# Attention scores in quarters of the TensorE array, and a value product split by key halves

## The chip, the cores and the metric

One core of a Trainium2 chip. The metric is the device time of one execution in microseconds, the median of several runs.

## The reference, cut to what matters

Three stages follow one another. The first is gated linear attention for 4 sequences of 768 positions, 8 heads of 48 numbers; the second a top-2 mixture of 8 experts on the 3072 rows it gives; the third a gated two-layer block on all rows. Only the first is touched:

```
f = sigmoid(f_logit)
for t in range(768):
    state = f[t][:, None] * state + outer(k[t], v[t])   # per head, 48 x 48
    y[t] = q[t] @ state
```

## The kernel before

**Tiles.** The 3072 positions are 24 tiles of 128, worked on in 12 pairs, tiles a and b of a pair k. The tiles 0 to 5 are the first sequence, 6 to 11 the second, and so on. Within a tile the recurrence is turned into a causal product: y = (masked scores) times v, plus what the state brought from the tile before gives. The state is carried from tile to tile in a sequence; after the last tile of a sequence (the b of the pairs 2, 5, 8 and 11) there is none.

**Scores by levels.** Decay between a key and a query is worked in by six levels. Level 0 takes blocks of 4 positions, the levels 1 to 5 blocks of 8, 16, 32, 64 and 128, of which only the part with keys in the left half of a block and queries in its right half is new. `scores(t, n)` (L1827) computes level n of tile t on TensorE into the bank pair pA[t % 2]: for each of the 4 pairs of heads c, two matmuls, one for each head s, with the head's 64 rows as contraction, the tile's keys (128, later 112, 96, 64) as stationary columns and all 128 queries as moving columns. What isn't new is computed and thrown away. Then VectorE multiplies the scaled keys and queries W by products of decays in `double_blocks(t, n)` (L1315), which the next level's scores need. The new scores are taken to SBUF, into aT: levels 0 to 2 by VectorE, `take_masked` (L1338, a copy under a mask, over 1024 and then 512 elements a partition); levels 3 to 5 by ScalarE, `take_rect` (L985, rectangular blocks).

**Value product.** `attend(t, cs)` gives y of a tile: when a state is inherited, four matmuls of 128 by 128 (L1881) with it, then eight matmuls aT times v with all 128 keys (L1886). `turn_keys` (L1864) transposes the keys for the state, `key_values` (L1901) multiplies them with v, `turn_x` (L1911) transposes y, `logit_parts` (L1924), `logits` (L1934) and `ranks` (L1946) begin the routing of the second stage.

**Queues.** Every engine executes a queue written by hand, a `body(k)` for each pair. In body k TensorE computes the scores of pair k and the value products of pair k - 1 (tiles a - 2 and b - 2); other engines work on pair k + 1 too. The parts of the queues that matter here, in order:

- TensorE: the body that the diff shows.
- ScalarE: take_rect(b - 2, 5), take_logit_parts, take_keys(a - 2), take_keys(b - 2) unless b - 2 ends a sequence (L994, reads what turn_keys left), inner_decays(k + 1) (L963, L965), soft_noise (L1030 to L1038), take_y(a - 2) (L1000), decay_factors(k + 1) (L973, L974), spread_state(a - 2) (L1007), take_x(a - 2), take_rect(a, 3), take_rect(b, 3), take_y(b - 2), take_rect for level 4 and (a, 5), spread_state(b - 2), take_x(b - 2).
- GpSimd: decay_state(a - 2), add_noise (L767), clamp(k + 2) (L709), merge_inner(k + 1) (L719), turn_first for both tiles of pair k + 1 (L727, L728), products(k + 1) (L739, L744), decay_state(b - 2) (L752), four scatters (L776).
- VectorE: double_blocks(b - 2, 5), to_block_ends(b) (L1293), take_masked(a, 0), take_masked(b, 0), double_blocks(a, 1), take_masked(a, 1), take_ranks (L1433, waits for ranks and logits) and take_rows, double_blocks(b, 1), take_masked(b, 1), double_blocks(a, 2), take_masked(a, 2), new_state(a - 2) (L1347 or L1350), double_blocks(b, 2), take_masked(b, 2), top2 (L1385), double_blocks(a, 3), turn_others(a + 2) (L1283), double_blocks(b, 3), turn_others(b + 2), double_blocks(a, 4), two small steps, new_state(b - 2) (needs decay_state(b - 2)), double_blocks(b, 4), to_block_ends(a + 2), a small step, double_blocks(a, 5).

After the pairs, TensorE goes on to the experts (L2041, L2073) and the last stage (L2152). The first expert's weights are loaded by the sync queue once the last pair but one has its key_values(b - 2) (through load_v and its waits), and cast by ScalarE (L1055) in the middle of body 11.

## Time and profile before

| | |
|---|---|
| median of 3 runs | 1233.04 us (1231.67 to 1234.83) |
| span of the profiled execution | 1221.6 us |
| TensorE busy (matmul) | 1185.8 us, 97% of the span |
| VectorE, ScalarE, GpSimd busy | 687.1, 481.6, 479.4 us |
| attention pairs | from 0 to about 284 us |

The span is counted from the first to the last instruction; the profile gives no time of its own for what lies around it in that execution, and the median of the runs is 11.4 us above its span. The busy time of matmuls is modelled, so 97% doesn't say that TensorE is at its peak. A matmul on 32-bit data shows as two records.

### The profile page before, as it was taken

To read this page: it belongs to the slowest core of one execution; us is meant where nothing else is said; L and a number is where in the kernel's file an instruction comes from. 1 tells how busy PE (TensorE), PEld (TensorE's weight loads), DVE (VectorE), ACT (ScalarE), POOL (GpSimd) and SP (SyncE) were. 2 spreads that over 40 slices of the span, in tenths; PEclk is the share of its full clock that TensorE was granted. 3 is DMA by queue.
4 is the path that set the end of the run, shared out by engine and by line. 5 is a ranking of instruction groups with operands and counts; after the bars stand their busy time and mean duration, and the time that the engine had idled before them with its cause. 6 is when DMAs were issued, how large, how long until landed. Compare 5 with 4: busy or idle time off the path is not lost.

```text
span 1221.6 us, 25186 instructions
## 1 busy us (share of the span) xinstructions
PE 1185.8 (97%) x8085; PEld 1037.9 (85%) x8086; DVE 687.1 (56%) x1215; ACT 481.6 (39%) x968; POOL 479.4 (39%) x463
## 2 busy tenths in 40 slices
PE   4999999999999999999999999999999999999998
PEld 4777787788888999999999998888888888888887
DVE  7888988887534454544444554445445454454433
ACT  4666665556333343433333443332322323223212
POOL 8458777754573617163357552220020200100000
PEclk9999999999999999999999999999999999999999
DMA  6233343343577868687788864130030301201000
GB/s 229 72 112 122 123 140 101 109 167 124 188 234 236 250 199 260 202 255 224 237 248 267 248 221 145 52 104 27 28 77 26 104 27 45 60 26 52 27 1 26
DMA packets 109523, 164.78 MB, mean 135 GB/s; under 512 B 48384, under 2 KB 85504, under 8 KB 108928
## 3 DMA queue, kind: packets, MB, share of 16 engines
q1 hardware_dynamic: 97584, 115.48, 30.5%
q0 software_dynamic: 11712, 47.98, 12.6%
q8 instruction: 53, 0.87, 0.3%
q14 instruction: 30, 0.25, 0.1%
q10 hardware_dynamic: 144, 0.20, 0.0%
HBM read 107.45 MB, written 56.16 MB: 134 GB/s over the span
## 4 chain that ended last, share of the span: by engine, by line
PE 82%; POOL 6%; DVE 4%; issue 3%; ACT 2%; DMA 2%; SPq 0%; DVEq 0%; POOLq 0%; ACTq 0%
PE pD L2041 17%; PE pD L2152 12%; PE pA L2152 12%; PE pA L2073 9%; PE pS L2073 9%; PE pA L2180 6%; PE pA L1850 5%; PE pX L2180 3%; PE pS L2180 3%; DVE W L1315 1%; POOL qk L728 1%; POOL fT L709 1%; POOL prods L744 1%; DMA stage<-w 1%; POOL qk L727 1%
## 5 line engine op out<-in xcount | busy, mean ns | idle before, releaser
L2041 PE MATMUL pD<-we,xsH 128*128 x612 | 189.6, 391 | 0.1
L1850 PE MATMUL pA<-W 64*128 64x128 f32 (+3 forms) x1920 | 136.8, 283 | 15.7 <-DVE W L1315 12.2
L1763 DVE TENSOR_TENSOR gs<-pD,sig 128x512 f32<-128x512 f32 x71 | 49.1, 692 | 169.3 <-ACT sig L1229 169.3
L1850 PEld LDWEIGHTS pA<-W 64*128 64x128 f32 (+3 forms) x1920 | 112.7, 170 | 34.8 <-DVE W L1315 18.7
L948 POOL DMA_INDIRECT pair<-y_sorted,y_row x40 | 38.8, 970 | 248.9 <-DMA z_rows<-pair 229.5
L2041 PEld LDWEIGHTS pD<-we,xsH 128*128 128x128 f32 x612 | 114.1, 188 | 22.2 <-issue 0.5
L2041 PE MATMUL pD<-we,xsL 128*128 x306 | 120.1, 392 | 0.0
L1229 ACT ACTIVATE sig<-pD 128x512 f32<-128x512 f32 x71 | 42.6, 600 | 192.4 <-PE pA L2152 192.4
L1315 DVE TENSOR_TENSOR W<-W,prods 128x512 f32<-128x512 f32 (+1 forms) x120 | 101.9, 856 | 22.9 <-PE pA L1850 20.8
L2073 PE MATMUL pA<-we,hidH 128*128 (+1 forms) x448 | 114.5, 336 | 0.0
L1495 DVE STREAM_TRANSPOSE pA<-hidP 128x512 f32<-128x512 f32 x98 | 64.6, 705 | 81.5 <-DMA hidP<-hid_rows 81.3
L2073 PE MATMUL pS<-we,hidH 128*128 x416 | 106.1, 336 | 0.4 <-ACT yo L1136 0.4
L1128 ACT ACTIVATE hidH<-pA 128x512 fp32r<-128x512 f32 x110 | 65.1, 599 | 95.0 <-DVE pA L1495 91.4
L837 POOL TENSOR_TENSOR we<-stage,we 128x1536 fp32r<-128x1536 f32 x28 | 98.6, 3521 | 0.6
L1487 DVE STREAM_TRANSPOSE pX<-xs 128x384 f32<-128x384 f32 x50 | 35.6, 712 | 104.4 <-DMA xs<-x_sorted 104.2
L1122 ACT ACTIVATE hid<-pD 128x512 f32<-128x512 f32 x100 | 59.9, 600 | 82.9 <-PE pD L2041 74.3
L2152 PE MATMUL pA<-zH,valL 128*128 128x512 f32 x216 | 85.9, 399 | 0.0
L2152 PE MATMUL pD<-zH,gateL 128*128 128x512 f32 x216 | 85.9, 399 | 0.0
L2152 PE MATMUL pD<-zH,gateH 128*128 128x512 f32 x216 | 85.6, 398 | 0.0
L1235 ACT CAST uH<-u 128x512 fp32r<-128x512 f32 x71 | 44.1, 620 | 105.3 <-DVE u L1766 103.8
L2152 PE MATMUL pA<-zH,valH 128*128 128x512 f32 x216 | 84.8, 394 | 0.0
L2152 PE MATMUL pA<-zL,valH 128*128 128x512 f32 x216 | 84.4, 392 | 0.0
(315 smaller groups left out, 2660.9 us busy)
## 6 DMA issues: line engine op xcount, KB each, us to landing
hid_rows<-hid SPq DMA_DIRECT2D x49, 512.0 KB, 3.4
hidP<-hid_rows SPq DMA_DIRECT2D x196, 128.0 KB, 2.9
stage<-w POOLq DMA_DIRECT2D x48, 384.0 KB, 4.7
qk<-qk_t SPq DMA_DIRECT2D x24, 512.0 KB, 3.7
y_sorted<-yo SPq DMA_DIRECT2D x53, 192.0 KB
xs<-x_sorted SPq DMA_DIRECT2D x200, 48.0 KB, 2.1
fT<-f_t SPq DMA_DIRECT2D x12, 512.0 KB, 4.2
vN<-v_n SPq DMA_DIRECT2D x24, 256.0 KB, 2.7
```

The source lines that it names most:

```text
L837: return pool.tensor_tensor(low, src, high.bitcast(F32), ALU.subtract)
L1122: act.activation(to, fr, ACT.Relu).then_inc(s_relu, 1)
L1128: act.activation(hidH[t.par][:, h * HF:(h + 1) * HF], pA[0][:, h], ACT.Relu).then_inc(s_hh, 1)
L1235: act.copy(uH[f % 2][:], u[f % 2][:]).then_inc(s_uh, 1)
L1315: dve.tensor_tensor(half[:, used], half[:, used], other[:, used], ALU.mult).then_inc(s_upd[t % 2], 1)
L1495: dve.transpose(pA[0][:, h].rearrange("p (k j t) -> p k j t", k=k, j=Q), hidP.rearrange("p (j k f) -> p k j f", j=Q, k=FC)[:, h * k:(h + 1 ...
L1763: dve.tensor_tensor(gs[:], pD[:, f % 2 * 512:f % 2 * 512 + TT], sig[f % 2][:], ALU.mult).then_inc(s_u, 1)
L1850: ins = pe.matmul(pA[par][keys, s, c * P:(c + 1) * P], both[r, 1, c, keys], both[r, 0, c], start=True, stop=True)
L2041: ins = pe.matmul(hidden_bank(t, h), (xsL if a else xsH)[t.par][:, k * P:(k + 1) * P], we[:, bass.ds(at + (b * WE + k * F + h * HF), HF)], ...
L2073: ins = pe.matmul(y_bank(t), (hidL if a else hidH)[t.par][:, k * P:(k + 1) * P], we[:, bass.ds(at + ((2 + b) * WE + k * DM), DM)], start=k ...
L2152: ins = pe.matmul(bank, (low if b else high)[:, c:c + P], (zL if a else zH)[t.par][:, k * TT:(k + 1) * TT], start=n == 0, stop=n == len(or ...
L2180: ins = pe.matmul(out_bank(j), (uL if a else uH)[f % 2][:, j * P:(j + 1) * P], outL[:, f * DM:(f + 1) * DM] if b else high[:, at * DM:(at ...
```

## The change

The scores of a level are no longer computed with 128 queries for all keys. For levels 0 to 4 each head gets two matmuls, left keys by left queries and right keys by right queries, 64 by 64 each, so four quarters of the array (two heads by two key halves) are addressed with 64 moving columns. Level 5 has left keys by right queries alone. A head's scores now take 64 columns in PSUM, and take_masked reads half as many elements. The two tiles' scores of a level stand next to each other in TensorE's queue. The value product is cut in three: `inherit` (the state's part, now eight matmuls of 64 output rows), `attend_late` (late keys, by late queries only; it needs level 4 at most) and `attend` (the first 64 keys, all queries). turn_keys(b - 2), ranks and logits come after attend(a - 2). The masks get three more copies at the start on GpSimd. The queues of the other engines keep their order.

```diff
...
 
 def block_masks(pool, mask, done):
 
+    lower = slice(HS, P)
     for l, h in enumerate(SMALL):
         v = mask[:, l * HP * HS:(l + 1) * HP * HS].rearrange("p (c b u) -> p c b u", c=HP, u=h)
         nb = P // (2 * h)
         pool.affine_select(out=v, in_=v, pattern=[[0, HP], [-2 * h, nb], [0, h]], compare_op=ALU.is_ge,
                            fill=0.0, base=0, channel_multiplier=1).then_inc(done, 1)
-        pool.wait_ge(done, 2 * l + 1)
+        pool.wait_ge(done, 3 * l + 1)
         pool.affine_select(out=v, in_=v, pattern=[[0, HP], [2 * h, nb], [0, h]], compare_op=ALU.is_ge,
                            fill=0.0, base=h - 1, channel_multiplier=-1).then_inc(done, 1)
-        pool.wait_ge(done, 2 * l + 2)
+        pool.wait_ge(done, 3 * l + 2)
+        pool.tensor_copy(v[lower, :, 0:nb // 2], v[lower, :, nb // 2:]).then_inc(done, 1)
+        pool.wait_ge(done, 3 * l + 3)
     n = len(SMALL)
     v = mask[:, n * HP * HS:].rearrange("p (b u) -> p b u", u=BASE)
 
     pool.affine_select(out=v, in_=v, pattern=[[-BASE, P // BASE], [0, BASE]], compare_op=ALU.is_ge,
                        fill=0.0, base=0, channel_multiplier=1).then_inc(done, 1)
-    pool.wait_ge(done, 2 * n + 1)
+    pool.wait_ge(done, 3 * n + 1)
     pool.affine_select(out=v, in_=v, pattern=[[BASE, P // BASE], [1, BASE]], compare_op=ALU.is_ge,
                        fill=0.0, base=0, channel_multiplier=-1).then_inc(done, 1)
+    pool.wait_ge(done, 3 * n + 2)
+    pool.tensor_copy(mask[lower, n * HP * HS:n * HP * HS + HS],
+                     mask[lower, n * HP * HS + HS:n * HP * HS + P]).then_inc(done, 1)
+    pool.wait_ge(done, 3 * n + 3)
 
 
 def halves_of(pair, h):
...
                 h = LEVELS[n - 1]
                 for b in range(P // (2 * h)):
                     left = slice(2 * h * b, 2 * h * b + h)
-                    right = slice(2 * h * b + h, 2 * h * (b + 1))
-                    ins = act.copy(aT[t % 4][left, :, :, right],
-                                   pA[t % 2][left].rearrange("p s (c n) -> p s c n", c=HP)[:, :, :, right])
+                    at = 2 * h * b % HS + h
+                    fr = pA[t % 2][left, :, 0:HP * HS].rearrange("p s (c n) -> p s c n", c=HP)
+                    if n < NL:
+                        fr = fr[:, :, :, at:at + h]
+                    ins = act.copy(aT[t % 4][left, :, :, at:at + h], fr)
                 ins.then_inc(s_rect[t % 2], 1)
 
             def take_keys(t):
...
                 i = t // 2
                 dve.wait_ge(s_a[t % 2], FILLS * i + n + 1)
                 if n == 0:
-                    dve.wait_ge(s_cs, 2 * MASKED)
+                    dve.wait_ge(s_cs, 3 * MASKED)
                     if t >= 4:
                         dve.wait_ge(s_y, t - 3)
                 else:
                     dve.wait_ge(s_lev[t % 2], MASKED * i + n)
+                to = aT[t % 4][:, :, :, 0:HS].rearrange("p a c b -> p (a c) b")
+                fr = pA[t % 2][:, :, 0:HP * HS].rearrange("p a (c b) -> p a c b", b=HS)
                 if n:
                     h = LEVELS[n - 1]
-                    to = aT[t % 4].rearrange("p a c (b s u) -> p a (c b) s u", s=2, u=h)[:, :, :, 1]
-                    fr = pA[t % 2].rearrange("p a (b s u) -> p a b s u", s=2, u=h)[:, :, :, 1]
+                    to = to.rearrange("p m (b s u) -> p m b s u", s=2, u=h)[:, :, :, 1]
+                    fr = fr.rearrange("p a c (b s u) -> p a c b s u", s=2, u=h)[:, :, :, :, 1]
                     at = (n - 1) * HP * HS
-                    mk = mask[:, at:at + HP * HS].rearrange("p (b u) -> p b u", u=h)
-                    mk = mk.unsqueeze(1).to_broadcast([P, 2, HP * HS // h, h])
+                    mk = mask[:, at:at + HP * HS].rearrange("p (c b u) -> p c b u", c=HP, u=h)[:, 0, 0:HS // (2 * h)]
+                    mk = mk.unsqueeze(1).to_broadcast([P, H, HS // (2 * h), h])
                 else:
-                    to = aT[t % 4].rearrange("p a c b -> p (a c) b")
-                    mk = mask[:, len(SMALL) * HP * HS:].unsqueeze(1).to_broadcast([P, H, P])
-                    fr = pA[t % 2].rearrange("p a (c b) -> p (a c) b", b=P)
+                    at = len(SMALL) * HP * HS
+                    mk = mask[:, at:at + HS].unsqueeze(1).to_broadcast([P, H, HS])
                 dve.copy_predicated(to, mk.bitcast(I32), fr).then_inc(s_lev[t % 2], 1)
 
             def new_state(t):
...
                     else:
                         pe.wait_ge(s_rect[par], RECTS * i + n - MASKED)
                 both = W[t % 6] if n else qk[t % 4]
+                left, right = slice(0, HS), slice(HS, P)
+                blocks = ((left, right),) if n == NL else ((left, left), (right, right))
                 for c in range(HP):
-                    for s in range(2):
-                        r = slice(HS * s, HS * (s + 1))
-                        keys = slice(0, P - LEVELS[n - 1] if n >= MASKED else P)
-                        ins = pe.matmul(pA[par][keys, s, c * P:(c + 1) * P], both[r, 1, c, keys], both[r, 0, c],
-                                        start=True, stop=True)
+                    for keys, asks in blocks:
+                        for s in range(2):
+                            r = slice(HS * s, HS * (s + 1))
+                            ins = pe.matmul(pA[par][keys, s, c * HS:(c + 1) * HS], both[r, 1, c, keys],
+                                            both[r, 0, c, asks], start=True, stop=True)
                 ins.then_inc(s_a[par], 1)
 
             def turn_keys(t):
...
                     ins = pe.transpose(pX[:, c * P:(c + 1) * P], W[t % 6][:, 1, c], ident[:])
                 ins.then_inc(s_kt, 1)
 
-            def attend(t, cs):
+            def inherit(t):
 
                 pe.wait_ge(s_upd[t % 2], NL * (t // 2 + 1))
-                pe.wait_ge(s_rect[t % 2], RECTS * (t // 2 + 1))
+                pe.wait_ge(s_yt, t)
+                pe.wait_ge(s_spread, states_up_to(t - 1))
+                for c in range(HP):
+                    for s in range(2):
+                        pe.matmul(pD[HS * s:HS * (s + 1), c * P:(c + 1) * P], stateB[1 - t % 2][:, c, s],
+                                  W[t % 6][:, 0, c], start=c == 0, stop=False, skip_group_check=True)
+
+            def attend_late(t):
+
+                pe.wait_ge(s_rect[t % 2], RECTS * (t // 2) + RECTS - 1)
                 pe.wait_ge(s_v[t % 4], 16 * (t // 4 + 1))
                 if t == 0:
                     pe.wait_ge(s_clear, 1)
                 else:
                     pe.wait_ge(s_yt, t)
-                inherits = not first_of_sequence(t)
-                if inherits:
-                    pe.wait_ge(s_spread, states_up_to(t - 1))
-                if inherits and cs[0] == 0:
-                    for c in range(HP):
-                        pe.matmul(pD[:, c * P:(c + 1) * P], stateB[1 - t % 2][:, c].rearrange("p s d -> p (s d)"),
-                                  W[t % 6][:, 0, c], start=c == 0, stop=False, skip_group_check=True)
-                for c in cs:
-                    y = pD[:, c * P:(c + 1) * P]
+                late = slice(HS, P)
+                for c in range(HP):
                     for s in range(2):
-                        ins = pe.matmul(y[HS * s:HS * (s + 1)], vN[t % 4][:, 2 * c + s], aT[t % 4][:, s, c],
-                                        start=not inherits, stop=True, skip_group_check=True)
-                if cs[-1] == HP - 1:
-                    ins.then_inc(s_y, 1)
+                        ins = pe.matmul(pD[HS * s:HS * (s + 1), c * P + HS:(c + 1) * P], vN[t % 4][late, 2 * c + s],
+                                        aT[t % 4][late, s, c, 0:HS], start=first_of_sequence(t) and c == 0,
+                                        stop=False, skip_group_check=True)
+                ins.then_inc(s_late, 1)
+
+            def attend(t):
+
+                pe.wait_ge(s_rect[t % 2], RECTS * (t // 2 + 1))
+                pe.wait_ge(s_late, t + 1)
+                soon = slice(0, HS)
+                for c in range(HP):
+                    for s in range(2):
+                        ins = pe.matmul(pD[HS * s:HS * (s + 1), c * P:(c + 1) * P], vN[t % 4][soon, 2 * c + s],
+                                        aT[t % 4][soon, s, c], start=False, stop=True, skip_group_check=True)
+                ins.then_inc(s_y, 1)
 
             def key_values(t):
 
...
                 now, old = is_pair(k), is_pair(p)
                 if now:
                     scores(a, 0)
+                    scores(b, 0)
                 if old:
                     turn_keys(a - 2)
+                    if not first_of_sequence(a - 2):
+                        inherit(a - 2)
                 if now:
-                    scores(b, 0)
+                    scores(a, 1)
+                if old:
+                    attend_late(a - 2)
+                if now:
+                    scores(b, 1)
+                if old:
+                    attend(a - 2)
                 if old and not last_of_sequence(b - 2):
                     turn_keys(b - 2)
-                if now:
-                    scores(a, 1)
                 if is_pair(k - 3):
                     ranks(k - 3)
                 if is_pair(k - 2):
                     logits(k - 2)
                 if old:
-                    attend(a - 2, (0,))
-                if now:
-                    scores(b, 1)
-                if old:
-                    attend(a - 2, (1, 2, 3))
+                    key_values(a - 2)
                 if now:
                     scores(a, 2)
-                if old:
-                    key_values(a - 2)
-                if now:
                     scores(b, 2)
                 if old:
                     turn_x(a - 2)
+                    inherit(b - 2)
                 if now:
                     scores(a, 3)
                 if old:
-                    attend(b - 2, (0,))
+                    attend_late(b - 2)
                 if now:
                     scores(b, 3)
                 if old:
-                    attend(b - 2, (1, 2, 3))
-                if now:
-                    scores(a, 4)
+                    attend(b - 2)
                 if old and not last_of_sequence(b - 2):
                     key_values(b - 2)
                 if now:
+                    scores(a, 4)
                     scores(b, 4)
-                if now:
-                    scores(a, 5)
                 if old:
                     turn_x(b - 2)
                 if now:
+                    scores(a, 5)
                     scores(b, 5)
                 if old:
                     logit_parts(p)
...
             turn_keys(a)
             ranks(NP - 3)
             logits(NP - 2)
-            attend(a, (0,))
+            inherit(a)
+            attend_late(a)
             turn_rows(Tile(0))
-            attend(a, (1, 2, 3))
+            attend(a)
             key_values(a)
             hidden(Tile(0))
             pe.wait_ge(s_xl, 1)
             turn_x(a)
-            attend(b, (0, 1, 2, 3))
+            inherit(b)
+            attend_late(b)
+            attend(b)
             turn_hidden(Tile(0))
             logit_parts(NP - 1)
             turn_x(b)
```

## Rows read from the trace of the kernel before

**Rows 1.** The page: busy time of TensorE, and the chain by engine.

```profile
PE 1185.8 (97%) x8085; PEld 1037.9 (85%) x8086; DVE 687.1 (56%) x1215; ACT 481.6 (39%) x968; POOL 479.4 (39%) x463
...
PE 82%; POOL 6%; DVE 4%; issue 3%; ACT 2%; DMA 2%; SPq 0%; DVEq 0%; POOLq 0%; ACTq 0%
```

**Rows 2.** Busy time by stretch of 30 us (from:to, length, engines).

```profile
150.00:180.00 30.00, 28.89 (x394) 24.13 (x392) 26.14 (x54) 18.55 (x44) 21.51 (x27) 1.00 0.46 143
...
330.00:360.00 30.00, 30.00 (x154) 26.95 (x153) 9.43 (x15) 9.58 (x19) 26.12 (x18) 1.00 0.70 200
```

**Rows 3.** Groups of instructions by line, 60 to 330 us.

```profile
L1850 PE MATMUL pA<-W 64*128 64x128 f32 (+3 forms) x1584 | 112.0, 281 | 10.8 <-DVE W L1315 9.6 <-DVE aT L1338 1.1
...
L1338 DVE COPY_PREDICATED aT<-mask,pA 128x512 f32<-128x512 int32 (+1 forms) x58 | 51.5, 895 | 0.9 <-PE pA L1850 0.9
```

**Rows 4.** Timeline of TensorE (start, length, what): logit_parts, right behind scores(b, 5).

```profile
54.63 0.64 PE L1924 MATMUL pD<-yT,wr 128*32 128x256 f32 x8
...
77.79 0.64 PE L1924 MATMUL pD<-yT,wr 128*32 128x256 f32 x8
...
100.78 0.64 PE L1924 MATMUL pD<-yT,wr 128*32 128x256 f32 x8
...
123.81 0.64 PE L1924 MATMUL pD<-yT,wr 128*32 128x256 f32 x8
...
147.31 0.64 PE L1924 MATMUL pD<-yT,wr 128*32 128x256 f32 x8
...
169.79 0.64 PE L1924 MATMUL pD<-yT,wr 128*32 128x256 f32 x8
```

**Rows 5.** The chain, 99.8 to 122.8 us (start, length, what).

```profile
99.83 1.02 PE pA L1850 x16
...
104.19 0.60 PE pX L1864 x4
...
104.81 0.59 ACT kEnd L994
...
108.18 0.23 POOL rsp L767
...
121.18 0.47 POOL stateD L752
...
122.05 0.69 DVE W L1315
```

**Rows 6.** The chain in pair 10, where TensorE alone carries it.

```profile
245.14 0.37 PE pD L1886 x4
245.51 1.09 PE pA L1850 x16
246.60 0.81 PE pD L1886 x12
...
248.50 0.60 PE pS L1901 x16
```

**Rows 7.** Timeline of VectorE, 122 to 169 us.

```profile
126.22 2.48 DVE L1338 COPY_PREDICATED aT<-mask,pA 128x1024 f32<-128x1024 int32 x2
...
162.30 1.16 DVE L1315 TENSOR_TENSOR W<-W,prods 128x512 f32<-128x512 f32 x1
...
167.38 0.71 DVE L1315 TENSOR_TENSOR W<-W,prods 128x512 f32<-128x512 f32 x1
```

**Rows 8.** Timeline of the start: TensorE and GpSimd.

```profile
12.90 2.08 PE L1850 MATMUL pA<-qk 64*128 64x128 f32 x16 [12.90 <-POOL qk L728]
...
9.51 1.04 POOL L719 TENSOR_TENSOR FG<-FG 128x512 f32<-128x512 f32 x1 [1.64 <-ACT FG L974]
```

**Rows 9.** The chain at the end of the pairs.

```profile
258.72 12.03 DMA stage<-w
```

**Rows 10.** Between the stages: timeline of TensorE, then its busy time and granted clock.

```profile
762.35 1.09 PE L2192 MATMUL pX<-ident,z_first 128*128 128x128 f32 x4 [2.14 <-DVE z_first L1784]
...
763.00:764.00 1.00, 1.00 (x6) 0.50 0.00 0
```

More of the change, by code:

```diff
@@ L365, in program @@
         s_y = sem("s_y")
+        s_late = sem("s_late")
         s_yt = sem("s_yt")
```

## The prediction

> **What bounds the kernel now.** I read the page first: TensorE is busy 97% and holds 82% of the chain [rows 1]. That is an average over stages, so I cut the span by time. In the expert stages TensorE is busy 30.00 us of 30; in the attention pairs it is 28.89 and VectorE 26.14, so neither is simply the bound [rows 2]. The change touches only the pairs, up to some 284 us. There the scores cost 112.0 us of TensorE and the masked copies 51.5 us of VectorE [rows 3]: both get cheaper, and that is the tempting sum. So I looked at what closes the loop from pair to pair. The end of a pair is its logit_parts: the pairs 2 to 6 take 23.16, 22.99, 23.03, 23.50 and 22.48 us [rows 4]. The chain of pair 4 [rows 5] is to be read as a ring: scores(b, 5) at 99.83, then TensorE up to the end of turn_keys(b - 2) at 104.79, ScalarE (take_keys, inner_decays, soft_noise) to 108.18, GpSimd from add_noise through clamp, merge, turn_first and products to decay_state, ending at 121.65, VectorE (new_state, double_blocks(b, 4)) to 122.74, and TensorE's next scores(b, 5). 4.96 + 3.4 + 13.5 + 1.1 = 23.0 us. Where tile b - 2 has a state to pass on (pairs 1, 2, 4, 5, 7, 8) this ring sets the period; where it has none (pairs 3, 6, 9) TensorE and VectorE do, hand in hand.
>
> **What a matmul costs.** In [rows 6] twelve records take 0.81 us and four take 0.37: the eight more are four slots of two heads, 0.11 us a slot, and 0.15 us is left, which I read as the change from one shape of the array to another. With 64 stationary and 48 moving columns sixteen records take 0.60: less 0.15, 0.056 a slot. Quarters of 64 by 64 with 64 moving columns never ran. If all four of a group share a slot, scores take 8 x 0.058 = 0.46 us, 0.61 with a change of shape, against 1.09. If only two quarters run at a time it is 16 x 0.058 + 0.15 = 1.08. I take the first: two row halves share a slot in the scores of before, two column halves in attend. No row shows both at once; the bounds are 0.46 and 1.08.
>
> The Trainium skill (TensorE: Matmul & The Clock Gate, on the back-to-back issue gap) has matmuls start no closer than some 25 ns. By that the 32 records of a quartered score would take 0.8 us in place of 0.46. No row here shows small quarters; the sum does without it.
>
> **The change part by part.**
>
> *TensorE.* inherit: eight matmuls of two records, 8 x 0.11 + 0.15 = 1.03, as before. attend_late: new, 8 x 0.058 = 0.46 between scores of the same shape. attend: 0.88 + 0.15 with its change, less 0.15 where scores of the same shape precede: 0.88. Two tiles' scores together: 0.92 + 0.15 = 1.07. A pair's work on TensorE falls by some 12 x 0.5 - 0.9 = 5 us.
>
> *VectorE.* The level 0 copy goes from 1024 to 512 elements, 1.24 [rows 7] to about 0.7 (the mixed mean of both sizes is 0.895 [rows 3]), the others from 0.7 to 0.4: 2 x 0.6 + 4 x 0.3 = 2.4 us a pair.
>
> *Where turn_keys(b - 2) goes.* It now stands behind scores(a, 1), attend_late, scores(b, 1) and attend of a - 2. Behind it in ScalarE's queue stand take_keys(b - 2), inner_decays, soft_noise, take_y and decay_factors, and GpSimd's whole part of the ring waits for them. From scores(b, 5): 0.46, logit_parts 0.6, both level 0 scores 1.07, turn_keys(a - 2) 0.6, inherit 1.03, together 3.8 us. scores(a, 1) needs take_masked(a, 0): VectorE reaches it 3.5 us after double_blocks(b, 4) (126.22 [rows 7] less 122.74 [rows 5]) and needs 0.7, so it starts at 4.3. Then 0.46, 0.46, 0.46, 0.88 and turn_keys 0.6: 7.2 us against 4.96, 2.3 later. The GpSimd part shrinks from 13.5 to some 12.7, since decay_factors is then ready in time and VectorE's operations overlap it less (bounds 12.0 and 13.5). Ring: 7.25 + 3.4 + 12.7 + 1.1 = 24.45 us. Against before: pairs 4 and 7 +1.4 each, 2, 5 and 8 +1.1 each, together +6.1. Pair 1 has no soft_noise to wait for; its decay_factors was behind attend alone and is now behind turn_keys and inner_decays: +2.0.
>
> *Pairs 3, 6, 9.* No turn_keys(b - 2). attend ends at 6.6, ranks and logits at 7.6; take_ranks and take_rows now hold VectorE until 8.4, double_blocks and the copy of (b, 1) end at 9.5, (a, 2) and new_state at 11.3, spread_state at 12.0, inherit(b - 2) at 13.1, scores(a, 3) at 13.7. From there the old stretch of double_blocks and turn_others, 162.30 to 168.0 [rows 7], 5.7 us: 19.4 in place of 22.7. 3 x 3.3 = -9.9 us.
>
> *Filling, pair 0.* TensorE and VectorE alternate. The halved copies give 2.4 us, and some four waited-for scores 0.5 each, more while the first still take 2.08 [rows 8] (twice the 1.09 of later): -4.3. The mask copies: three short ones, nothing longer than GpSimd's affine steps of the same size, in the 1.64 us that GpSimd waits for ScalarE [rows 8]; hidden, and if the cover is gone they cost at most what exceeds it.
>
> *Pairs 10 and 11, and the end.* The load of the first expert starts behind key_values(b - 2) of pair 10 and takes 12.03 us [rows 9]; ScalarE waits for it in body 11. key_values comes 0.4 us sooner, and half of pair 11 behind that wait is shorter by 0.8: -1.2. Behind the pairs two attend_late (0.9) and VectorE's work, which no longer hides behind TensorE (0.8): +1.7.
>
> Without the clock: -4.3 + 6.1 + 2.0 - 9.9 - 1.2 + 1.7 = -5.6 us.
>
> *The clock.* TensorE has 5 us less to do in a ring that is 1 us longer. In the ring pairs its idle time gathers in two places: before inherit(b - 2), which waits for spread_state behind decay_factors (some 2.5 us), and before scores(b, 5) (some 3.5 us). The longest such gap in the pairs now is 1.4. What a longer one does, the trace shows once: TensorE sat idle for 2.14 us, and behind it the granted clock was 0.50, that is 1.2 GHz, until 766 us [rows 10], some 3.4 us. The gap before scores(b, 5) lies just ahead of the 7.2 us of the ring that are TensorE's. If the clock falls there, 2.6 us of path at full clock cost 1.3 more. Eight pairs (1, 2, 4, 5, 7, 8, 10, 11): +10.4. I take it, because both gaps are longer than the one that did it. Bounds: 0 and, if the whole 7.2 us ran slow, of which half is waiting for VectorE, 8 x 3 = 24.
>
> The Trainium skill (the same page, its table on why this matters) asks for no long idle gaps between bursts of matmuls, else the clock halves. By that the sum is 10.4 us above the one without gaps, as I took it from the rows; the trace agrees with its one fall.
>
> Sum: -5.6 + 10.4 = +4.8. The sum is made against the span of 1221.6, which becomes 1226.4; with the 11.4 us between span and median, 1238.
>
> **The rivals.**
>
> A. *The clock holds.* For it: a single fall in the trace, at a place where the matmuls before were of another kind; the gaps of 1.4 us did nothing. Then 1233.0 - 5.6 = 1227.4 us, faster. It decides if gaps of 2.5 and 3.5 us leave the clock at 2.4 GHz.
>
> B. *Quarters run two at a time.* Then scores cost as before: seven of a ring pair's stand on the path or in inherit's, and TensorE is the bound: +0.5 us for four scores in the ring (2.0 a pair, 8 pairs) and 2.5 in the others, some +24, while the busy TensorE keeps its clock (-10): 1252 us.
>
> C. *The ring isn't rigid.* GpSimd could make up the delay, if its part shrinks towards what its operations take alone and new_state isn't last. Then all pairs gain like 3, 6 and 9: 11 x 3.3 + 4.3 = 40 us less, 1193. Against it: at 121.65 VectorE starts new_state in the same tenth of a microsecond as decay_state ends [rows 5].
>
> **How the numbers follow.** Less than 0.3% (3.7 us) can't be told from no change here. Forecast (ring longer, clock falls) 45%, its own range 1230 to 1248; A 30%, 1220 to 1233; B 17%, 1243 to 1264; C 8%. From the forecast 0.30 lies above 1236.7, 0.15 within; A gives 0.08 within and 0.22 below; B is all slower, C all faster. Together slower 0.47, same 0.23, faster 0.30. From 1222 to 1256, C, the low end of A and the high end of B are left out, two in ten.
>
> **What would show it.** Ring: logit_parts to logit_parts 24 to 26 us in the pairs 1, 2, 4, 5, 7, 8, under 21 in 3, 6, 9. Scores: sixteen matmuls, 32 records, in about 0.5 to 0.6 us. take_keys(b - 2) ends 7 to 9 us behind scores(b, 5) instead of 5.6. Clock: below 1.00 in windows of the pairs. VectorE: copies at some 0.7 and 0.4 us. I'd be wrong if GpSimd's idle time before add_noise grew without the pair's period growing, or if scores stayed near 1.09.

## The result and the profile after

The changed kernel takes 1271.1 us (median; 1262.5 to 1273.9), the kernel before 1232.4 beside it: ratio 1.030, interval 1.028 to 1.033. The forecast was 1238, 1222 to 1256: the direction was right, the time lay outside the range. The profiled execution has a span of 1267.5 us, 46.0 more than before, and a mean granted clock of 0.957.

The page after: TensorE's busy time, its granted clock in the 40 slices, the instruction queue, the chain by engine.

```profile
PE 1174.8 (93%) x10549; PEld 1030.1 (81%) x10550; DVE 656.0 (52%) x1215; ACT 478.3 (38%) x968; POOL 483.7 (38%) x466
...
PEclk9886796888999999999999999999999999999999
...
q8 instruction: 72, 1.18, 0.4%
...
PE 75%; POOL 7%; issue 5%; DMA 5%; DVE 3%; ACT 3%; SPq 1%; DVEq 0%; POOLq 0%; ACTq 0%
```

TensorE is busy 11 us less than in [rows 1], though part of its work ran at half clock, and it waits more; every digit of the clock below 9 lies in slices 2 to 10, among the attention pairs. Windows of TensorE (columns as in [rows 2]):

```profile
150.00:180.00 30.00, 22.71 (x620) 19.61 (x622) 20.85 (x48) 17.52 (x47) 24.22 (x27) 0.89 0.27 99
...
101.00:108.00 7.00, 6.29 (x112) 4.72 (x116) 6.58 (x11) 1.95 (x5) 6.12 (x8) 0.51 0.03 11
108.00:111.40 3.40, 2.18 (x63) 1.64 (x64) 0.15 (x1) 0.54 (x1) 2.58 (x3) 1.00 0.42 164
111.40:125.00 13.60, 12.50 (x190) 11.04 (x187) 6.19 (x25) 6.68 (x15) 6.08 (x8) 0.50 0.36 114
```

The last row shows a whole pair's middle at 1.2 GHz: 13.6 us at 0.50. In all, 109 us of the first 345 are at half clock; in the kernel before none. The costliest group of the pairs, against [rows 3]:

```profile
L1863 PE MATMUL pA<-W 64*64 64x64 f32 x2880 | 88.0, 247 | 38.7 <-DVE W L1325 24.9 <-DVE aT L1349 7.6 <-issue 6.1
```

The scores of levels 1 to 5 take 88.0 us, part of them at half clock, where they took 112.0, and the idle time ahead of them has grown from 10.8 to 38.7 us. The logit_parts on the timeline, as in [rows 4]:

```profile
56.52 0.64 PE L1950 MATMUL pD<-yT,wr 128*32 128x256 f32 x8
...
81.75 1.08 PE L1950 MATMUL pD<-yT,wr 128*32 128x256 f32 x8
...
103.88 1.08 PE L1950 MATMUL pD<-yT,wr 128*32 128x256 f32 x8
...
133.81 1.08 PE L1950 MATMUL pD<-yT,wr 128*32 128x256 f32 x8
...
163.53 1.08 PE L1950 MATMUL pD<-yT,wr 128*32 128x256 f32 x8
...
185.43 0.64 PE L1950 MATMUL pD<-yT,wr 128*32 128x256 f32 x8
```

The same eight matmuls take 0.64 or 1.08 us: the second is the half clock at the end of pairs 2 to 5. The differences of such starts are the periods of the pairs, here for this and for later kernels (us; last column: us at half clock in the first 345):

| pair | 2 | 3 | 4 | 5 | 6 | 7 | 8 | 9 | 10 | 11 | half |
|---|---|---|---|---|---|---|---|---|---|---|---|
| before | 23.2 | 23.0 | 23.0 | 23.5 | 22.5 | 23.0 | 23.5 | 22.5 | 22.7 | 22.6 | 0 |
| after | 25.2 | 22.1 | 29.9 | 29.7 | 21.9 | 30.0 | 29.9 | 21.9 | 28.2 | 28.4 | 109 |
| fill | 24.4 | 21.3 | 29.8 | 26.7 | 22.0 | 29.1 | 27.1 | 22.1 | 28.5 | 30.4 | 61 |
| fill_more | 24.4 | 22.7 | 24.0 | 25.2 | 23.0 | 24.8 | 24.8 | 21.0 | 23.6 | 26.4 | 20 |
| keys_ranks_fill | 21.9 | 20.7 | 21.4 | 22.4 | 20.2 | 21.4 | 22.4 | 23.8 | 21.3 | 31.3 | 20 |
| quarters_old_order | 23.8 | 19.9 | 24.6 | 24.3 | 21.5 | 24.3 | 27.4 | 21.0 | 25.8 | 23.2 | 58 |
| quarters_old_order_fill | 22.0 | 21.0 | 23.3 | 21.6 | 21.3 | 21.6 | 22.0 | 20.7 | 20.6 | 22.6 | 3 |
| before_fill | 25.0 | 24.1 | 24.4 | 25.4 | 24.1 | 24.4 | 25.4 | 24.1 | 24.7 | 25.4 | 0 |
| before_wait | 24.1 | 23.3 | 22.8 | 26.1 | 23.5 | 22.8 | 24.5 | 26.0 | 25.4 | 24.3 | 14 |

The chain after, in pair 4, to be laid beside [rows 5]:

```profile
102.83 1.12 PE pA L1863 x16
103.95 1.01 PE pD L1950 x8
104.96 1.92 PE pA L1863 x64
106.88 1.04 PE pX L1877 x4
107.92 0.67 PE pA L1863 x32
...
112.71 1.69 PE pD L1913 x16
114.40 1.06 PE pX L1877 x4
115.48 0.59 ACT kEnd L1004
...
118.76 0.23 POOL rsp L775
...
131.16 0.47 POOL stateD L760
...
132.03 0.69 DVE W L1325
132.72 0.04 issue
132.77 1.12 PE pA L1863 x16
```

It is the forecast ring: scores(b, 5), TensorE to the end of turn_keys(b - 2), ScalarE, GpSimd, VectorE, scores(b, 5). But TensorE's part takes 115.46 - 102.83 = 12.6 us, where 7.2 were forecast. The rest is 3.3 + 12.9 + 1.1, as forecast.

### The profile page after: what moved, and what is told of

It reads as the page before. It is cut to its first block, busy times and chain, and to the rows that moved or that the text cites. A ratio compares the mean times of both kernels' runs of the same rounds, so it can differ in the third digit from the quotient of the medians.

```text
span 1267.5 us, 30091 instructions
## 1 busy us (share of the span) xinstructions
PE 1174.8 (93%) x10549; PEld 1030.1 (81%) x10550; DVE 656.0 (52%) x1215; ACT 478.3 (38%) x968; POOL 483.7 (38%) x466
## 3 DMA queue, kind: packets, MB, share of 16 engines
q0 software_dynamic: 11712, 47.98, 11.9%
## 4 chain that ended last, share of the span: by engine, by line
PE 75%; POOL 7%; issue 5%; DMA 5%; DVE 3%; ACT 3%; SPq 1%; DVEq 0%; POOLq 0%; ACTq 0%
PE pD L2066 14%; PE pA L2180 12%; PE pD L2180 12%; PE pA L2098 8%; PE pS L2098 7%; PE pA L2208 6%; PE pA L1863 4%; PE pX L2208 3%; PE pS L2208 3%; DMA hidP<-hid_rows 2%; DMA hid_rows<-hid 2%; DVE W L1325 1%; PE pD L1913 1%; POOL qk L736 1%; POOL prods L752 1%
## 5 line engine op out<-in xcount | busy, mean ns | idle before, releaser
L1863 PE MATMUL pA<-W 64*64 64x64 f32 x3456 | 107.1, 254 | 45.3 <-DVE W L1325 26.6
L1863 PEld LDWEIGHTS pA<-W 64*64 64x64 f32 x3456 | 88.8, 161 | 61.0 <-DVE W L1325 38.9
L2066 PEld LDWEIGHTS pD<-we,xsH 128*128 128x128 f32 x612 | 114.1, 188 | 23.2 <-issue 1.3
L1325 DVE TENSOR_TENSOR W<-W,prods 128x512 f32<-128x512 f32 (+1 forms) x120 | 92.5, 779 | 58.0 <-PE pA L1863 43.9
L2180 PE MATMUL pD<-zL,gateH 128*128 128x512 f32 x216 | 84.4, 392 | 0.0
```

The source lines that it names most:

```text
L1325: dve.tensor_tensor(half[:, used], half[:, used], other[:, used], ALU.mult).then_inc(s_upd[t % 2], 1)
L1863: ins = pe.matmul(pA[par][keys, s, c * HS:(c + 1) * HS], both[r, 1, c, keys], both[r, 0, c, asks], start=True, stop=True)
L2066: ins = pe.matmul(hidden_bank(t, h), (xsL if a else xsH)[t.par][:, k * P:(k + 1) * P], we[:, bass.ds(at + (b * WE + k * F + h * HF), HF)], ...
L2180: ins = pe.matmul(bank, (low if b else high)[:, c:c + P], (zL if a else zH)[t.par][:, k * TT:(k + 1) * TT], start=n == 0, stop=n == len(or ...
```

## The experiments

Theory 1: the order makes the ring longer, as forecast, and the clock takes the rest. Rivals: stalls in TensorE's supply of instructions (theory 2); the order costs all of it (theory 3).

**fill.** Dummy matmuls in two places of the ring pairs; they wait as scores(t, n) does until its PSUM is free.

```diff
+                    if now and not last_of_sequence(b - 2):
+                        fill(a, 3, 5)
                     inherit(b - 2)
...
+                    if old and not last_of_sequence(b - 2):
+                        fill(b, 5, 10)
                     scores(b, 5)
+            def fill(t, n, times):
...
+                for _ in range(times):
+                    pe.matmul(pA[par][:, 0, 0:P], ident[:], ident[:], start=True, stop=True)
```

> The changed kernel with matmuls added that do no useful work: five of 128 by 128 before inherit(b - 2) and ten before scores(b, 5), in the pairs whose tile b - 2 has a state to pass on, where TensorE waits anyway. Theory (ring and clock): the ring stays as it is, but TensorE stays at 2.4 GHz; ring pairs take about 24.6 us instead of 29.8, the mean granted clock is 0.99 or more, and the time is about 1233 us (1227 to 1240). Rival 1 (the new order of the queue alone makes the pair long and the clock costs little): 1265 us or more. Rival 2 (the small matmuls themselves, or fetching so many instructions, cost the time): 1270 us or more, since there are more instructions still.

Measured: 1264.1 us, ratio 1.027; a miss by 31 us. The half clock fell to 61 us and pairs 5 and 8 lost 3 us, pairs 4 and 7 little, since their clock still fell. Too few dummies to decide.

**full_new_order.** The new order with the scores, masks and copies of the kernel before.

> The new order of TensorE's queue and the value product by key halves, but with the scores of before: all 128 queries, masks and copies of before. Theory: TensorE is busy, so the clock holds (0.99 or more), but turn_keys(b - 2) ends 9.9 us behind scores(b, 5), so a ring pair takes about 27.5 us and the time is about 1262 us (1250 to 1275). Rival 1: the same. Rival 2 (small matmuls are the cost): near 1235 us.

Measured: 1266.6, ratio 1.030. The pairs 4, 5, 7 and 8 take 27.2, 26.9, 27.1 and 26.9 us with no half clock in them. The order and the value product in three parts cost some 4 us a ring pair when the scores are at full price.

**quarters_old_order.** All new matmuls, masks and copies, with the queue order of before (attend(a - 2, ...) replaced by inherit, attend_late and attend at its two places).

> All new matmuls, masks and copies, but TensorE's queue in the order of before (inherit and attend_late where attend of the first head pair stood). Theory: turn_keys(b - 2) ends 3.5 us behind scores(b, 5); the ring falls to about 21 us and TensorE is busy enough to keep its clock for the most part (0.98 or more): about 1207 us (1200 to 1222). Rival 1: faster too. Rival 2 (small matmuls are the cost): 1245 us or more.

Measured: 1239.7, ratio 1.007; a miss by 33 us. Without any new order the clock falls too, 58 us in all, and the cheaper matmuls give nothing.

**keys_ranks_early.** The changed kernel with both turn_keys side by side, and ranks and logits behind scores(a, 1).

```diff
                     turn_keys(a - 2)
+                    if not last_of_sequence(b - 2):
+                        turn_keys(b - 2)
                     if not first_of_sequence(a - 2):
                         inherit(a - 2)
```

> The changed kernel with three steps moved back: turn_keys(b - 2) right behind turn_keys(a - 2), ranks and logits right behind scores(a, 1). The adjacent scores stay. Theory: turn_keys(b - 2) ends 3.8 us behind scores(b, 5), the ring is about 21 us, and the gaps that slow the clock go: about 1208 us (1200 to 1225). Rival 1 (adjacent scores are what costs): 1250 us or more. Rival 2 (small matmuls are the cost): 1250 us or more.

Measured: 1246.5, ratio 1.013; a miss again, by 38 us, with 68 us at half clock. These two kernels lay 33 and 38 us above their expectations, with 58 and 68 us at half clock: the clock had to be tested by itself.

**fill_more.** As fill, with more dummies and in every pair.

```diff
-                    if now and not last_of_sequence(b - 2):
-                        fill(a, 3, 5)
+                    if now:
+                        fill(a, 3, 9 if not last_of_sequence(b - 2) else 4)
...
+                        fill(b, 4, 3 if not last_of_sequence(b - 2) else 5)
...
+                        fill(a, 5, 3 if not last_of_sequence(b - 2) else 4)
...
+                        fill(b, 5, 9 if not last_of_sequence(b - 2) else 4)
```

> The changed kernel with more dummy matmuls (128 columns, identity by identity, into PSUM that the next scores overwrite; they compute nothing that is used): behind the copy of level 3 of tile a 9 in pairs that follow a pair of the same sequence on the state chain and 4 in the others, ahead of scores(b,4) 3 and 5, ahead of scores(a,5) 3 and 4, ahead of scores(b,5) 9 and 4. Theory 1 (the clock alone makes the difference between the forecast period and the measured one): half-speed time falls from 109 us of the changed kernel to under 15 us, pairs 4, 5, 7, 8 take 24.5 to 25.5 us instead of 30, pairs 10 and 11 25 instead of 28.3, the whole 1238 to 1245 us. Theory 2 (the stalls in which TensorE's records are 0.4 us apart have a cause of their own, the supply of its instructions): the clock still falls in several pairs, they stay at 27 or above, and the whole is 1255 or more. Theory 3 (order costs 4 us a pair by itself, as with full-width scores): the clock holds and the pairs still take 27: 1255.

Measured: 1237.2, ratio 1.008 (1.007 to 1.010). Work was added and 34 us came back; by the ratios it is 27, since the kernel before took 1226.1 beside this run and 1232.4 beside the changed kernel. That lies at the lower edge of theory 1's range, with 20 us at half clock where under 15 were expected. Its chain in pair 4:

```profile
103.25 0.64 PE pA L1863 x16
...
106.52 0.69 PE pA L1863 x32
...
108.95 0.60 PE pX L1877 x4
109.57 0.58 ACT kEnd L1004
...
112.86 0.23 POOL rsp L775
...
125.53 0.47 POOL stateD L760
```

TensorE's part is 6.3 us instead of 12.6. The pairs 2, 4, 5, 7 and 8 take 24.4, 24.0, 25.2, 24.8 and 24.8: on average 24.6, at full clock in all five, where the forecast ring without the clock was 24.45. At the end of pair 7 the chain runs through the dummies themselves (2.21 us from 198.01 on), so 24.6 is rather too long for the ring.

**quarters_old_order_fill** (fill(b, 4, 3 or 4), fill(a, 5, 3 or 4), fill(b, 5, 6 or 4) in quarters_old_order) and **keys_ranks_fill** (the same and fill(a, 3, 5 or 3) in keys_ranks_early).

> All matmuls, copies and masks of the changed kernel in the order of the kernel before, with dummy matmuls (128 columns, nothing of them is used) ahead of scores(b,4), scores(a,5) and scores(b,5): 3 or 4, 3 or 4, 6 or 4 of them. Without them this order had 58 us at half clock and took 1239.7. Theory 1 (clock alone): the half-speed time falls under 10 us; each us at half clock costs about half a us of the matmuls in it, so 20 to 28 us come back: 1212 to 1222, faster than before. Theory 2 (instruction supply): stalls and half clock stay in pairs 4, 7 and 9: 1232 to 1242.

> The changed kernel with turn_keys(b-2) right behind turn_keys(a-2) and ranks and logits right behind scores(a,1), and dummy matmuls (nothing of them is used) behind the copy of level 3 of tile a and ahead of scores(b,4), scores(a,5), scores(b,5). Without them it took 1246.5 with 68 us at half clock. Theory 1 (clock alone): clock above 0.99, ring pairs 22.5 to 23.5, the others 20.3 to 21: 1212 to 1222. Theory 2 (instruction supply): pair 5 stays near 30, whole 1238 to 1248.

Measured: 1211.1, ratio 0.987 (0.985 to 0.990), and 1217.1, ratio 0.992. The first lies just under theory 1's range, the second within it. The first is the fastest kernel of this study: the change's matmuls are worth 1.3% once TensorE is kept busy, and 3% against the kernel before with the same dummies (before_fill, below). In its chain a tile's scores take what was forecast:

```profile
117.03 0.61 PE pA L1863 x16
117.64 0.57 PE pD L1950 x8
118.21 0.62 PE pA L1863 x32
118.84 0.60 PE pX L1877 x4
```

keys_ranks_fill has one pair of 31.3 us; its timeline and its windows there:

```profile
247.46 1.08 PE L1863 MATMUL pA<-qk 64*64 64x64 f32 x57
250.59 0.39 PE L1863 MATMUL pA<-qk 64*64 64x64 f32 x7 [2.05 <-issue]
```

```profile
250.80:267.90 17.10, 16.33 (x229) 14.49 (x222) 6.50 (x25) 6.43 (x13) 3.08 (x6) 0.50 0.34 120
268.00:275.00 7.00, 7.00 (x207) 6.32 (x207) 4.91 (x8) 4.19 (x14) 3.42 (x4) 1.00 0.30 117
```

In the midst of one block of scores TensorE stands still for 2.05 us without waiting for an engine, and behind it the clock is 0.50 for 17.1 us, with 13 records a microsecond instead of 30. A pause as in theory 2 comes first and half clock as in theory 1 follows; that the one brings the other is not shown. The only fall in the pairs of quarters_old_order_fill, at 107.6 us, also stands right behind such a pause, of 1.79 us.

**split_moving.** The kernel before with each score matmul cut in two, but for the last level (so levels 0 to 4; the expectation misnames them), to add instructions alone.

```diff
-                        ins = pe.matmul(pA[par][keys, s, c * P:(c + 1) * P], both[r, 1, c, keys], both[r, 0, c],
-                                        start=True, stop=True)
+                        for q in range(1 if n == NL else 2):
+                            asks = slice(0, P) if n == NL else slice(HS * q, HS * (q + 1))
+                            at = c * P + asks.start
+                            ins = pe.matmul(pA[par][keys, s, at:at + asks.stop - asks.start], both[r, 1, c, keys],
+                                            both[r, 0, c, asks], start=True, stop=True)
```

> The kernel before with each score matmul of levels 0 to 7 cut into two of 64 moving columns: same order, same weights loaded twice, same values, and over 2000 more TensorE instructions, as the change adds. The scores of a tile are expected at 1.0 to 1.3 us. Theory 1 (clock alone): as before where they cost the same, 1228 to 1236, no half clock; if a score of a tile rises to 1.3 us it is up to 0.2 x 16 a pair dearer: 1240 to 1250, with each pair longer by the same amount. Theory 2 (instruction supply): idle pieces of 0.4 us between groups of 4 to 6 TensorE records and waits on remote semaphores of VectorE of 3 to 5 us appear that the kernel before doesn't have, and the clock falls in those pairs: 1240 or more, with some pairs longer by 2 to 7 us and others by nothing.

Measured: 1340.0, ratio 1.093. A tile's scores took 2.05 us, not 1.0 to 1.3, so TensorE became the bound and the comparison with theory 2 is weak: no remote wait and no idle piece, but no fast bursts either. What it says of columns stands at the end.

**before_fill.** The control: the kernel before with the dummies of quarters_old_order_fill.

> The kernel before with the dummy matmuls of the run quarters_old_order_fill (13 or 12 of 128 columns a pair, nothing of them is used), so a control: what the dummies cost or give where the clock was full anyway. They stand on TensorE's stretch, of which only the two ring parts set the period. The clock theory, in which they do nothing but hold the clock: 0 to +0.7 us a pair (13 x 0.056 where TensorE's work is the limit), 1226 to 1234, ratio 1.000 to 1.006. If dummies helped in some other way than by the clock (by spacing out the stalls), this kernel would get faster too, below 0.997.

Measured: 1246.8, ratio 1.018 (1.016 to 1.019), 13 us above what was expected at most. The dummies cost 1.8 us a pair where the clock was full anyway, so what they brought in fill_more is net of a price. But the kernel before has no stalls either (no idle piece that waits for nothing, 30 to 345 us). So this control doesn't tell whether the dummies help by holding the clock alone or by keeping the stalls away too, and no run separates the two.

**keys_early_fill.** keys_ranks_fill with ranks and logits left where the change has them.

> The changed kernel with turn_keys(b-2) alone moved, right behind turn_keys(a-2) (ranks and logits stay behind), and dummy matmuls (nothing of them is used) that hold the clock. It asks which step of the ring the order lengthened. If it is the place of turn_keys(b-2), as forecast (2.5 us more of the ring): ring pairs at full clock 22 to 22.8 us against 24.4 of fill_more and 21.4 to 22.4 of keys_ranks_fill, whole 1215 to 1225. If the place of ranks and logits counts as much (they feed pick and the noise on VectorE, which stand in the ring), ring pairs stay at 23.5 or more: 1228 to 1236.

Measured: 1227.6, ratio 1.002. Pairs 4, 5, 7 and 8 take 23.2, 24.1, 23.4 and 24.1, between the two cases: against fill_more (average 24.7) the keys give 1.0 and, against keys_ranks_fill (21.9), ranks and logits 1.8 more. Each of these pairs has 3.4 us at half clock, which may be most of the 1.8. Pair 2 is at full clock in all three kernels and takes 24.4, 23.4 and 21.9: 1.0 for the keys (with a few dummies less), 1.5 for the logits (there are no ranks yet in pair 2). Its chain in keys_early_fill passes from attend through the logits (L1960, 59.13) to ScalarE's soft_noise (59.72) and GpSimd's add_noise (60.48). Both steps of the order lengthen a pair, and I had counted only the first.

**old_order_keys_fill.** quarters_old_order_fill with turn_keys(b - 2) straight behind turn_keys(a - 2).

> The run quarters_old_order_fill (1211.1, ratio 0.9874) with turn_keys(b-2) straight behind turn_keys(a-2) instead of behind scores(b,0). If the ring (scores(b,5), turn_keys(b-2), ScalarE's copy, GpSimd, VectorE) still sets every ring pair, its TensorE part gets shorter by scores(b,0), 0.5 to 0.6 us, in seven ring pairs: 1206 to 1209. If VectorE's level chain of the two tiles sets the period there (its waits for TensorE's scores are 24 us over the stage), scores(b,0) comes later by 0.6 us and the same is lost: 1210 to 1215.

Measured: 1214.5, ratio 0.991: no gain. In that kernel the ring no longer sets the period alone.

**before_wait.** The kernel before with one more wait.

```diff
                 if old:
+                    if now:
+                        pe.wait_ge(s_lev[1], MASKED * (b // 2 + 1))
                     turn_x(a - 2)
```

> The kernel before, every instruction and its order kept, with one more wait on TensorE: ahead of turn_x(a-2) it waits until VectorE and ScalarE have copied level 2 of tile b. By the trace of before this makes TensorE idle from 135.93 to 137.98, 2.05 us, in every pair from 2 on, of which later idle pieces (0.39 and 0.59 us) and the slack of the stretch can take back about 1. If an idle piece of 2 us is by itself enough to lose the clock: half clock appears in most pairs, 3 to 14 us each, none in the unchanged kernel, and the time is 20 to 60 us longer: 1246 to 1286; if the 0.4 us pieces and the remote waits come with the half clock and not from the number of instructions, they appear here too, with the instructions of the kernel before. If the clock falls in the changed kernel for another reason (quarters, more instructions), it stays at full here and each pair takes 1 us more at most: 1226 to 1237.

Measured: 1241.1, ratio 1.015 (1.011 to 1.020), between the two cases. Two of its eleven waits on the timeline, and three windows behind them:

```profile
93.92 0.65 PE L1911 MATMUL pX<-ident,yT 128*128 128x128 f32 x4 [2.10 <-DVE aT L1338]
...
140.62 0.65 PE L1911 MATMUL pX<-ident,yT 128*128 128x128 f32 x2 [2.10 <-DVE aT L1338]
```

```profile
94.00:98.00 4.00, 4.00 (x48) 3.36 (x48) 3.20 (x8) 1.51 (x5) 3.92 (x6) 1.00 0.02 4
...
140.70:144.10 3.40, 3.40 (x22) 2.82 (x23) 1.42 (x7) 0.84 (x3) 3.25 (x6) 0.50 0.00 0
144.20:148.00 3.80, 3.80 (x53) 3.20 (x54) 2.37 (x4) 2.02 (x9) 3.41 (x6) 1.00 0.02 4
```

The same 2.10 us of idle time are followed by full clock once and by half clock the other time; of eight idle pieces of 2.1 us three were, in pairs 5, 9 and 10 (the other three were of 1.4 to 1.5 us, and none of them was). So the clock can fall at such an idle piece, with no quarter and no instruction added, but does not always, and it stays low for 3.4 to 6.8 us. Pairs 5 and 8, which took 23.5 both before, take 26.1 with 3.4 us at half clock and 24.5 without: 1.6 us for 3.4. There are no 0.4 us stalls and no remote waits here.

**old_order_fill_less.** quarters_old_order_fill with 7 dummies a pair.

> The run quarters_old_order_fill (1211.1, ratio 0.9874, 3.4 us at half clock) with 7 dummy matmuls a pair instead of 13 or 12: 2 ahead of scores(b,4), 2 ahead of scores(a,5), 3 ahead of scores(b,5). The dummies cost the kernel before 1.7 us a pair. If fewer still hold the clock, 0.3 to 0.8 us a pair come back: 1203 to 1208. If the clock falls in some pairs, each us at half clock costs about 0.5: 20 us of it give 1215 to 1222.

Measured: 1211.8, ratio 0.988. Half the dummies, four falls of 3.4 us instead of one, and the time is between the two cases: what one gives the other takes.

## Why the prediction was wrong

The span grew by 46.0 us and not by 4.8. (Between the medians it is 38.7 us: the profiled execution of the kernel before lay 11.4 us under its median, that of the changed kernel 3.6, so some 7 us of the 46.0 come from which executions were profiled.) Where the 41.2 lie, from the starts of logit_parts:

| part | forecast | measured | missed |
|---|---|---|---|
| filling and pair 1 (-4.3 + 2.0 + 1.3) | -1.0 | +1.9 | 2.9 |
| pairs 2, 4, 5, 7, 8 (+6.1 + 5 x 1.3) | +12.6 | +28.5 | 15.9 |
| pairs 3, 6, 9 | -9.9 | -2.1 | 7.8 |
| pairs 10, 11 (-1.2 + 2 x 1.3) | +1.4 | +11.4 | 10.0 |
| end | +1.7 | +2.9 | 1.2 |
| expert stages and last stage | 0 | +3.4 | 3.4 |

*Scores and copies: right.* 0.61 to 0.62 us in the chain against the forecast 0.61; rival B is out. The Trainium skill (TensorE: Matmul & The Clock Gate, the back-to-back issue gap) lets matmuls start no closer than some 25 ns, from which the estimate was 0.8 us: 0.62 for 32 records is 19 ns each, so the measurement decides against that estimate for quarters. VectorE's copies, by their line:

```profile
L1349 DVE COPY_PREDICATED aT<-mask,pA x60: 416/430/740, 59.6 to 309.6; 128x256 f32<-128x256 int32 x40, 128x512 f32<-128x512 int32 x20
```

0.43 and 0.74 us, forecast 0.4 and 0.7.

*The ring: right in size, in part by luck.* It carries the chain, it is rigid (rival C is out), and at full clock it takes 24.6 us in fill_more against 24.45. But the forecast put the whole lengthening down to turn_keys(b - 2), of which keys_early_fill shows some 1.0 us; the logits, which it had not counted in the ring, make 1.5. Pair 2 of the changed kernel, whose TensorE part ran at full clock, has 7.5 us from scores(b, 5) to the end of turn_keys(b - 2), forecast 7.2.

*The clock: the mis-sized term, and the step that failed.* "If the clock falls there, 2.6 us of path at full clock cost 1.3 more" took one fall of 3.4 us a ring pair, as the one of [rows 10]. (As it is worded the sum doesn't come out: 2.6 us of path at full clock would cost 2.6 more. 1.3 is the price of 2.6 us spent at half clock.) With it TensorE's part of the ring would have been 7.2 + 1.3 = 8.5 us. Measured are 12.6, 11.9, 12.2 and 12.1 us in the pairs 4, 5, 7 and 8, some 5 us above 7.2 in each. Two things make them.

The first is the half clock itself: falls of 3.4 to 13.7 us, two in each of the ring pairs 2, 4, 5, 7 and 8, 109 us in all. In pairs 5 and 8, 9.4 and 9.7 us of TensorE's part ran at 0.50. Even the bound of 24 us (3 us a pair) was too low. The idle pieces were there (1.96 us before scores(b, 5) at 132.77, 2.44 and 3.11 us before others), shorter than the forecast 3.5. The mistake was to carry over the length of the only low stretch, which lies in another stage. Why the clock stays low for longer in the pairs is not shown: idle time alone doesn't explain it, since in the 13.6 us shown above TensorE was busy 12.50 us.

The second is a term that the sum did not have: stalls, idle pieces of some 0.4 us in which TensorE waits for nothing that the profile shows, in the pairs 4, 7, 10 and 11. They are shown under "What stays open". From scores(a, 1) to the end of turn_keys(b - 2) pair 4 takes 7.5 us and pair 7 takes 8.0, against 3.0 in fill_more (from 106.52 to 109.55). Of these 4.5 and 5.0 us some 1.2 are half clock on attend and turn_keys; the other 3.3 and 3.8 are the stalls and the short pieces between them, at full clock for the most part. All idle pieces that wait for nothing add up to 11.0 us between 30 and 345 us in the changed kernel, to 2.9 in fill_more and to none in the kernel before.

Together: the four pairs 4, 5, 7 and 8 take 29.9 on average, with 15.1 us at half clock, and 24.7 in fill_more, 5.2 us a pair, 0.34 for each microsecond at half clock with the stalls counted in. Over 109 us that is an estimate of 37, against the 10.4 in the sum: some 27 of the 41 missed, for clock and stalls together and rough in size. The Trainium skill (TensorE: Matmul & The Clock Gate, on why this matters) asks for no long idle gaps between bursts; this case agrees in part: in before_wait it is a risk at each gap and not a rule, and split_moving lost the clock with no gap at all.

*Pairs 3, 6, 9: forecast too short by 1 us or more, clock or not.* Forecast 19.4. In the changed kernel pairs 6 and 9 take 21.9 with 2.5 and 2.7 us at half clock. Half clock can cost at most half of its own length, here 1.4 us, so 20.5 is left. The fill kernels of the new order agree, with 20.2 (keys_ranks_fill) and 21.0 (fill_more, pair 9) at the shortest. So less than two thirds of the expected 3.3 us was there, and the clock took part of that.

*The filling* had 10.2 us at half clock before 50 us, which the sum did not have at all, and its gain of 4.3 was eaten: the first logit_parts starts at 56.52, against 54.63 before. In keys_ranks_early, with full clock up to there, it starts at 52.05.

*What stays open.* 3.4 us in the stages behind the pairs. And stalls that appear after and not before: pieces in which TensorE runs five or six records and stops.

```profile
109.68 0.35 PE L1863 MATMUL pA<-W 64*64 64x64 f32 x4
110.43 0.35 PE L1863 MATMUL pA<-W 64*64 64x64 f32 x5 [0.40 <-issue]
111.18 0.36 PE L1863 MATMUL pA<-W 64*64 64x64 f32 x6 [0.41 <-issue]
111.95 0.76 PE L1863 MATMUL pA<-W 64*64 64x64 f32 x17 [0.41 <-issue]
```

They stand ahead of the 13.6 us at half clock, while the clock is still 1.00, and also at 190, 272 and 313 us: the first three times in the dense run of quarters behind turn_keys(a - 2), the last time behind inherit(b - 2). In the chain of pair 7 the stretch from scores(a, 1) to the end of turn_keys(b - 2), with the stalls of 190 us in it, goes from the first of these lines to the end of the second:

```profile
189.01 0.69 PE pA L1863 x32
...
195.99 1.06 PE pX L1877 x4
```

Waits of VectorE and ScalarE on no engine of the core appear as well:

```profile
DVE W L1325 <- remote: 14.2, 4, 5.2
...
ACT aT L996 <- remote: 5.2, 1, 5.2
```

Such waits occur in after, fill, full_new_order, quarters_old_order and keys_ranks_early, which have 17 to 109 us at half clock; all of these but full_new_order also have the stalls in series. Neither the waits nor the series occur in the kernels with more instructions still but enough dummies, nor in split_moving with 68 us at half clock. So neither the added instructions nor the half clock make them alone. Whether the stalls are late instructions that low clock and idle time bring about, or the other way round, no run settles.

## What to carry to other kernels

Making TensorE's work cheaper in a loop whose period another chain sets turns it into idle time, and this idle time can cost the clock: here matmuls worth 1.3% ended, by the new order, the clock and the stalls, as a loss of 3%. Read the granted clock in windows of one period, not on the page; and before moving or shaving anything test the kernel with dummy matmuls where the gaps would be, which separates the order from the rest if there are enough of them (those of fill were too few), and run the kernel before with them too, for their price. Where a step is moved behind others, count every consumer that it feeds: here the places of turn_keys and of ranks and logits each cost a ring pair one to two microseconds.

## What the hardware showed

- Halving the moving columns alone saves nothing. In split_moving:

```profile
116.82 2.05 PE L1853 MATMUL pA<-W 64*128 64x64 f32 x32
```

  32 records (two to a matmul) of 64 moving columns with 128 stationary ones take 2.05 us, 16 with 128 moving columns take 1.02 to 1.09 [rows 5, 6]; 32 of quarters (64 stationary, 64 moving) take 0.62.
- The clock can fall with TensorE busy all the time. In split_moving, no idle time at all around it:

```profile
221.00:229.00 8.00, 8.00 (x117) 7.03 (x115) 4.63 (x5) 3.68 (x6) 0.17 (x1) 1.00 0.12 45
...
231.00:265.00 34.00, 34.00 (x313) 30.79 (x314) 12.04 (x27) 9.61 (x24) 15.29 (x22) 0.50 0.23 75
```

  34 us at 0.50, twice in the run, at a price of some 15 us each (pairs 7 and 10 take 44.5 and 44.7, the others 28.5 to 30.1). What brings it on is not known.
- The instruction queue moved 72 packets of 16 KB after, as the page shows above, against 53 before: in the pairs mostly one every 4 to 7 us instead of 8 to 11. One of them, 1.5 us long, lies at 110.7 us, within the stalls shown from 109.7 on, and others at 191.0 and 272.8 us, within two of the other series; in the series at 313 us there is none. fill_more moved 76 and has no such series, so the number of packets alone doesn't make them.
